# Pooled attention feeding two expert stages on one Trainium2 core: the order of the score chunks, the shape of the minimum over scores, and the visits of the product with v

## The chip, the cores and the metric

The kernel runs on one core of one Trainium2 chip. The metric is device time in microseconds (us). The core's engines work side by side and meet at semaphores: TensorE (PE in the profile, with its weight loads shown apart as PEld), VectorE (DVE), ScalarE (ACT), GpSimd (POOL) and SyncE (SP), which issues most of the transfers.

## The reference

Three parts follow each other. Only the first, attention, is touched by the change.

```python
q_pool = q.reshape(B, H, S // 2, 2, D).mean(axis=3)       # B, H, S, D = 4, 8, 1152, 64
scores = scale * np.matmul(q_pool, k.transpose(0, 1, 3, 2))
scores = scores - np.max(scores, axis=-1, keepdims=True)
attn = np.exp(scores)
attn = attn / (np.sum(attn, axis=-1, keepdims=True) + 1e-09)
attn_out = np.matmul(attn, v)                              # then to (B*S/2, H*D) = x
```

Then x goes through a soft mixture of 8 experts with 4 slots each (logits x @ phi, softmax over tokens and over slots, two products per expert with a relu between), and last through h = x @ w_in, (h - tanh(h)) @ w_out. All inputs and the output are float32.

## The kernel before

**Pairs, rounds and tiles.** The 32 heads are worked in 16 pairs (`over_pairs`; the first two and last two pairs are written out, the 12 between run in a hardware loop). A pair has 576 pooled query rows for each of its two heads. They make nine tiles of 128 rows in five rounds: rounds 0, 1, 3 and 4 work a tile of each head (double rounds), and round 2 (`MIX`) works one tile that holds the last 64 rows of both heads.

**A round.** `scores` makes the scores of a tile against 1152 keys in three chunks, of 512, 512 and 128 keys (chunks 0, 1, 2), in this order. Each chunk takes three products (high and low halves of split operands) for each head, and lies in PSUM bank 3 * head + chunk, so banks 0 to 5 hold a round's scores. Scores are made with a negative factor, so their minimum is the wanted maximum. On VectorE `maximum` takes it, head after head: a reduction over each 512-wide chunk, then one `tensor_scalar` with an accumulated minimum over the 128-wide chunk, which takes the two reduced values as scalars. ScalarE's `exponential` waits for that, and writes one probability row block of 1152 columns in one instruction. TensorE turns (transposes) it in nine 128-wide pieces (`turn_prob`), and ScalarE and VectorE copy the turned pieces to `probT` (`evac`). Head 0's turned chunks use banks 0, 1 and 2, head 1's use banks 6, 5 and 4. VectorE copies head 0's chunk 1 (`second_a`) and both heads' chunk 2 (`third_evac`); ScalarE copies both heads' chunk 0 (`first_evac`) and head 1's chunk 1 (`second_b`).

**The order on TensorE** in each round: the three chunks of scores, each behind the waits of `banks_free`; in round 2 also the turning of the next pair's k and q (`turn_k_and_q`); in rounds 1 and 3 the turning back of an output (`turn_out`); a visit of the product with v; the turning of head 0; perhaps a second visit; the turning of head 1. The product with v (`pv`) of a group of query tiles has 18 matmuls in the program, each of which shows as two in the profile. `PV_AT` gives each visit as (round, place): (group, pairs back, from, to). Group 0 has 320 columns and group 1 has 256.

**Round 2 to round 3.** Round 2 turns the next pair's k and q into banks 3 to 6. VectorE copies k out (`k_raw`, L432), ScalarE copies q out (`q_raw`, L500), and GpSimd makes the high and low parts. In the code before, ScalarE first copies chunk 0 of the mixed tile and then q. Round 3's first scores wait for chunk 0 of the mixed tile to be copied (`first_evac`) and for `k_copied`; its second chunk waits for `second_a` and `third_evac`; its third waits for `q_evac`.

**Downstream.** SyncE prefetches expert weights during the last pair; one of these transfers goes to memory that the attention's operands of the odd pairs use, so it waits for the last scores.

Of the kernel before, what the change touches and what calls it, by code (L numbers as in the profile page):

```python
# [10 lines left out]
P = 128  # L11
# [6 lines left out]
def attention(nc, dram, sizes, sb, x, ident, rep, rep_ready, rep_step, early, prefetch):  # L18
# [19 lines left out]
    def heads_of(r):  # L38
        return 1 if r == MIX else 2

    def tiles_of(p, r):

        return p * TILES + 2 * r - (1 if r > MIX else 0)
# [5 lines left out]
    def group_of(r):  # L49
# [3 lines left out]

    PV_AT = {(3, 0): (0, 0, 0, 8), (3, 1): (0, 0, 8, 10), (4, 0): (0, 0, 10, 18),
             (0, 0): (1, 1, 0, 10), (0, 1): (1, 1, 10, 12), (1, 0): (1, 1, 12, 18)}
    OUT_AT = {1: 0, 3: 1}
    PV_EVAC_AT = {0: 0, 2: 1}

    with ExitStack() as ctx:
# [19 lines left out]
        part_neg = sb("part_neg", [P, 2, 2])  # L79
        spare = sb("spare", [P, P])  # L80
        neg_max = sb("neg_max", [P, TILES])
# [55 lines left out]
        def _(sp):  # L137
# [33 lines left out]
            over_pairs(sp, body)  # L171
            sp.wait_ge(scores_full, PAIRS * ROUNDS * NCH)
            prefetch(sp, 2)
# [49 lines left out]
        def turned(h, c):  # L223

            n = (CHUNK[c][1] - CHUNK[c][0]) * P
            return ps[:, (c, (TBANK, 5, 4)[c])[h], 0:n]

        @block.tensor
        def _(pe):
# [27 lines left out]

            def banks_free(p, r, c, first, last):

                before = tiles_of(p, r)  # L260
                if c == 0:
                    wait(pe, first_evac, before - (0 if r == MIX + 1 else 1))
                    if r == MIX + 1 and not last:
                        pe.wait_ge(k_copied, p + 1)
                elif c == 1:
                    wait(pe, second_a, p * ROUNDS + r)
                    wait(pe, third_evac, before)
                elif r == MIX + 1 and not last:
                    pe.wait_ge(q_evac, p + 1)
                elif r != MIX:  # L270
                    wait(pe, second_b, doubles_of(p, r))

# [41 lines left out]
            def body(p, par, first, last):  # L314
                for r in range(ROUNDS):
                    for c in range(NCH):
                        banks_free(p, r, c, first, last)
                        if r == 0 and c == 0:
                            if first:
                                pe.wait_ge(first_kl, 1)  # L320
                                pe.wait_ge(first_ql, 1)
                            wait(pe, k_low, p)
                            wait(pe, q_low, p)
                        scores(p, par, r, c)

                    wait(pe, first_evac, tiles_of(p, r))
                    if r == MIX and not last:
                        wait(pe, second_b, doubles_of(p, r))
                        turn_q_rest(p + 1, ps[:, TBANK - 1, BANK - P:BANK])
                        turn_k_and_q(p + 1, q_row)  # L330
                    if r in OUT_AT and not first:
                        turn_out(p - 1, OUT_AT[r])
                    visit(p, par, r, 0, first)
                    turn_prob(p, r, 0)
                    visit(p, par, r, 1, first)
                    if r != MIX:
                        if r in OUT_AT and not first:
                            pe.wait_ge(out_evac, (p - 1) * 2 + OUT_AT[r] + 1)
                        turn_prob(p, r, 1)
# [6 lines left out]

            def visit(p, par, r, n, first):
                if (r, n) in PV_AT:
                    g, back, lo, hi = PV_AT[r, n]
                    if not (back and first):  # L350
                        pv(p - back, par ^ back, g, lo, hi)
# [21 lines left out]
        def _(dve):  # L373
# [7 lines left out]

            def maximum(p, r, h):

                tau = tiles_of(p, r) + h
                j = tiles_of(0, r) + h
                full = (p * ROUNDS + r) * NCH
                part = part_neg[:, h]
                wait(dve, neg_done, tau - 1)
                for c in range(2):
                    dve.wait_ge(scores_full, full + c + 1)  # L390
                    nc.vector.tensor_reduce(part[:, c:c + 1], ps[:, 3 * h + c, :], AX.X, ALU.min).then_inc(part_done, 1)  # L391
                dve.wait_ge(scores_full, full + NCH)
                dve.wait_ge(part_done, tau * 2 + 2)
                wait(dve, exp_done, tau - TILES + 1)
                nc.vector.tensor_scalar(spare[:], ps[:, 3 * h + 2, 0:P], part[:, 0:1], part[:, 1:2],  # L395
                                        ALU.min, ALU.min, accum_out=neg_max[:, j:j + 1]).then_inc(neg_done, 1)

            def invert(p, par):
# [21 lines left out]
            def body(p, par, first, last):  # L420
                for r in range(ROUNDS):
                    tau = tiles_of(p, r)
                    for h in range(heads_of(r)):
                        maximum(p, r, h)
                    if r == 0 and not first:
# [23 lines left out]
        def _(act):  # L449
# [35 lines left out]
            def body(p, par, first, last):  # L485
                for r in range(ROUNDS):
# [3 lines left out]
                    for h in range(heads_of(r)):  # L490
                        exponential(p, par, r, h)
                    group_free(act, p, r)
                    act.wait_ge(ptr_full, tau * NCH + 1)
                    evac(copy, r, 0, 0).then_inc(first_evac, 1)
                    if r == MIX:
                        if not last:
                            act.wait_ge(qtr_full, p + 2)
                            act.wait_ge(k_copied, p + 1)
                            wait(act, q_low, p)
                            nc.scalar.activation(q_raw[:], q_row, ACT.Copy, scale=EXP_SCALE).then_inc(q_evac, 1)  # L500
                    else:
                        act.wait_ge(ptr_full, tau * NCH + NCH + 1)
# [587 lines left out]
def program(nc, dram, out, sizes):  # L1090
# [9 lines left out]
    def rows(start, *items):  # L1100

        table = {}
        for name, size in items:
# [4 lines left out]
    KV, QT, QR = S // P, SQ // P, SQ % P  # L1108
    QC = 2 * QT * P + 3 * QR
    XW = B * H // 2 * (QT + 1) * P  # L1110
# [9 lines left out]
               ("q_both", 2 * QT * D), ("q_both_r", 2 * D), ("q_raw", SQ + QR)),  # L1120
        **rows(ODD, ("kT0", 2 * S), ("qT_hi0", QC), ("qT_lo0", QC)),
        **rows(EVEN, ("kT1", 2 * S), ("qT_hi1", QC), ("qT_lo1", QC)),
        **rows(TOP, ("v_nat0", 2 * KV * D), ("v_nat1", 2 * KV * D), ("prob0", S), ("prob1", S), ("probT0", G0W), ("probT1", G1W),
               ("outT0", 2 * P + QR), ("outT1", 2 * P), ("ones", 8), ("warm", 8), ("part_neg", 8), ("spare", P), ("neg_max", 16),
               ("row_sum0", 16), ("row_sum1", 16), ("mix_sum0", 8), ("mix_sum1", 8), ("row_den", 16), ("row_inv", 16)),
# [12 lines left out]
    TABLE = {**NEVER, **ATTENTION, **KEPT, **GATING, **EXPERTS}  # L1138
    assert KEPT["stand"] + 32 <= PT and GATING["xT1"] + KD * SQ * 4 <= PT and GATING["row"] + 16 * NT <= END + 2048
    assert max(GATING["dT"] + LW * 4, ATTENTION["row_inv"] + 64) <= nc.sbuf_usable_end - BASE  # L1140
# [90 lines left out]
```

## Time and profile before

| | |
|---|---|
| median of three runs | 919.76 us (919.64 to 921.55) |
| the profiled execution's own time | 917.36 us |
| its span in the profile | 915.6 us |
| attention | from the start to 584 us |
| weight transfers, gating and experts | 584 to about 680 us |
| last part (w_in, tanh, w_out) | about 680 us to the end |
| PE busy over the span | 817.7 us (89%) |
| DVE, ACT, POOL busy | 551.7 us, 487.3 us, 248.7 us |

The span is that of the recorded instructions; the rest of the own time, 1.8 us, lies around it. Matmuls are pipelined and the ends of their rows are modelled, so a busy PE isn't PE at its peak. What sets the pace of the attention is read from the order in time within one round.

### The profile page before, as it was taken

How to read it: one execution, taken by the hardware profiler on the slowest of the kernel's cores; microseconds unless marked ns; L12 is line 12 of the kernel's file. 1: busy time of each engine (PE TensorE's matmuls, PEld its weight loads, DVE VectorE, ACT ScalarE, POOL GpSimd, SP SyncE). 2: the span in 40 equal slices, each digit the busy share in tenths (PEclk: the TensorE clock that was granted, in tenths of full speed). 3: DMA queues.
4: the chain of work that ended last, by engine and by line, in shares of the span. 5: the costliest groups of instructions: out<-in, count | busy, mean ns of one | idle time of the engine just before them, and what ended most of it. 6: DMA issues, size and time to landing. Idle time of an engine off the chain costs nothing. (4 is left out here: it accounts for less than half of the span.)

```text
span 915.6 us, 16591 instructions
## 1 busy us (share of the span) xinstructions
PE 817.7 (89%) x5819; PEld 595.7 (65%) x5819; DVE 551.7 (60%) x1112; ACT 487.3 (53%) x729; POOL 248.7 (27%) x154
## 2 busy tenths in 40 slices
PE   4899899899899898898899898878578999999998
PEld 3666666666666666666666666544235888888886
DVE  3666666666766666667667666350007667766673
ACT  2555565555555555555655654321019666666662
POOL 2304304304214124124034030000008544443333
PEclk9999999999999999999999999989989999999999
DMA  5343203213113023023023061707990000000000
GB/s 129 140 126 78 61 20 78 48 30 77 30 48 77 15 63 77 1 76 77 0 77 78 1 236 67 276 2 291 395 401 15 24 24 23 23 23 23 23 22 24
DMA packets 82161, 75.50 MB, mean 82 GB/s; under 512 B 42448, under 2 KB 60880, under 8 KB 81616
## 3 DMA queue, kind: packets, MB, share of 16 engines
q1 hardware_dynamic: 79792, 74.47, 25.6%
q10 hardware_dynamic: 2336, 0.59, 0.3%
q8 instruction: 21, 0.34, 0.2%
q14 instruction: 12, 0.10, 0.0%
HBM read 70.32 MB, written 4.72 MB: 82 GB/s over the span
## 5 line engine op out<-in xcount | busy, mean ns | idle before, releaser
L478 ACT ACTIVATE prob<-ps,neg_max 128x1152 f32<-128x1152 f32 x144 | 175.8, 1221 | 213.4 <-DVE spare L395 213.4
L280 PE MATMUL ps<-ident,prob 128*128 128x128 f32 x1296 | 174.6, 281 | 51.4 <-ACT prob L478 49.9
L391 DVE TENSOR_REDUCE part_neg<-ps 128x1 f32<-128x512 f32 x288 | 191.8, 688 | 46.2 <-PE ps L254 37.3
L280 PEld LDWEIGHTS ps<-ident,prob 128*128 128x128 f32 x1296 | 140.8, 142 | 107.0 <-ACT prob L478 97.9
L296 PE MATMUL ps<-probT,v_nat 128*64 128x256 f32 (+1 forms) x1152 | 160.5, 414 | 0.0
L363 DVE COPY probT<-ps 128x128 f32<-128x128 f32 (+1 forms) x192 | 75.5, 421 | 101.9 <-PE ps L280 101.9
L451 ACT ACTIVATE probT<-ps 128x512 f32<-128x512 f32 x208 | 116.8, 593 | 33.8 <-PE ps L280 33.8
L208 POOL TENSOR_TENSOR kT<-k_raw,ones 128x1152 fp32r<-128x1152 f32 x15 | 31.6, 2107 | 342.4 <-DVE k_raw L432 342.4
L254 PE MATMUL ps<-kT,qT_hi 64*128 64x512 f32 (+1 forms) x768 | 111.7, 366 | 4.8 <-DVE qT_lo L380 2.6
L296 PEld LDWEIGHTS ps<-probT,v_nat 128*64 128x64 f32 x1152 | 74.5, 136 | 51.2 <-issue 10.9
L948 PE MATMUL ps<-w_hi,g_even 128*128 128x512 f32 x320 | 102.7, 392 | 2.2 <-POOL g_even L1032 2.0
L254 PEld LDWEIGHTS ps<-kT,qT_hi 64*128 64x128 f32 x768 | 68.8, 187 | 29.5 <-issue 7.8
L948 PE MATMUL ps<-w_hi,g_odd 128*128 128x512 f32 x256 | 81.7, 390 | 0.0
L1006 ACT ACTIVATE slot<-ps 128x1024 f32<-128x1024 f32 x36 | 37.0, 1028 | 64.7 <-PE ps L932 64.7
L948 PEld LDWEIGHTS ps<-w_hi,g_even 128*128 128x128 f32 x320 | 60.2, 188 | 15.7 <-POOL g_even L1032 2.9
L254 PE MATMUL ps<-kT,qT_lo 64*128 64x512 f32 (+1 forms) x384 | 69.6, 354 | 0.0
L395 DVE TENSOR_SCALAR_CACHE_REDUCE spare<-ps,part_neg 128x128 f32<-128x128 f32 x144 | 59.0, 409 | 17.1 <-DVE part_neg L391 0.6
L1071 DVE SCALAR_TENSOR_TENSOR slot<-slot,ps 128x1024 f32<-128x1024 f32 x36 | 44.0, 1222 | 38.7 <-ACT ps L1008 38.7
L1032 POOL TENSOR_TENSOR g_even<-slot,g_even 128x1024 fp32r<-128x1024 f32 x20 | 48.2, 2408 | 58.1 <-ACT g_even L993 58.1
L948 PE MATMUL ps<-w_lo,g_even 128*128 128x512 f32 x160 | 62.6, 391 | 0.0
L1078 DVE COPY_PREDICATED slot<-slot,ps 128x1024 f32<-128x1024 uint32 x36 | 49.3, 1368 | 21.9 <-DVE slot L1071 20.3
L948 PEld LDWEIGHTS ps<-w_hi,g_odd 128*128 128x128 f32 x256 | 48.2, 188 | 9.7
(142 smaller groups left out, 1002.9 us busy)
## 6 DMA issues: line engine op xcount, KB each, us to landing
slot<-in_moe_w SPq DMA_DIRECT2D x16, 2048.0 KB, 12.8
v_nat<-in_v SPq DMA_DIRECT2D x16, 576.0 KB, 4.8
k_nat<-in_k SPq DMA_DIRECT2D x30, 288.0 KB, 4.0
q_nat<-in_q SPq DMA_DIRECT2D x32, 256.0 KB, 4.2
out<-res SPq DMA_DIRECT2D x18, 256.0 KB, 2.0
slot<-in_moe_w_in SPq DMA_DIRECT2D x2, 2048.0 KB, 20.7
slot<-in_moe_w_out SPq DMA_DIRECT2D x8, 512.0 KB, 16.8
q_nat_r<-in_q SPq DMA_DIRECT2D x32, 32.0 KB, 3.6
```

The costliest lines, as they stand in the source:

```text
L254: last = nc.tensor.matmul(ps[:, 3 * h + c, 0:k1 - k0], q[par][HALF[h], at], kT[par][HALF[h], part, k0:k1], start=(n == 0), stop=(n == 2))
L280: last = nc.tensor.transpose(dst[:, n * P:(n + 1) * P], prob[h][:, kt * P:(kt + 1) * P], ident[:])
L296: last = nc.tensor.matmul(ps[64 * h:64 * h + D, VBANK, 0:n], v_nat[par][:, h, kt, :], probT[g][:, kt, h, :], start=(kt == 0), stop=(kt == ...
L363: return copy(probT[g][:, k0:k1, h, col:col + P], src.rearrange("p (c q) -> p c q", c=n))
L391: nc.vector.tensor_reduce(part[:, c:c + 1], ps[:, 3 * h + c, :], AX.X, ALU.min).then_inc(part_done, 1)
L395: nc.vector.tensor_scalar(spare[:], ps[:, 3 * h + 2, 0:P], part[:, 0:1], part[:, 1:2], ALU.min, ALU.min, accum_out=neg_max[:, j:j + 1]).th ...
L451: return nc.scalar.activation(dst, src, ACT.Copy)
L478: nc.scalar.activation(prob[h][:], row, ACT.Exp, bias=neg_max[:, j:j + 1], scale=-1.0, accum_out=sums).then_inc(exp_done, 1)
L948: last = nc.tensor.matmul(ps[:, 2 * HB + i, :], a[par][:, ft * CW + i * P:ft * CW + (i + 1) * P], w(ft), start=(ft == 0 and k == 0), stop= ...
L1032: nc.gpsimd.tensor_tensor(g_block(g_lo, par, b), g[b % 2], g_block(g_hi, par, b).bitcast(F32), ALU.subtract).then_inc(gl_done, 1)
L1071: nc.vector.scalar_tensor_tensor(tv[b % 2], sq[b % 2], 1.0, h_of(b), ALU.subtract, ALU.mult).then_inc(series_done, 1)
L1078: nc.vector.copy_predicated(tv[b % 2], big[b % 2].bitcast(mybir.dt.uint32), th).then_inc(tanh_done, 1)
```

## The change

The short chunk of the scores is made first, before the two wide ones (`SCORE_ORDER`). On VectorE the minimum of a double round becomes: one short reduction for each head over its 128-wide chunk, one reduction over head 0's chunk 0, one `tensor_scalar` with accumulated minimum over head 0's chunk 1, and one over head 1's chunks 0 and 1 together, 1024 columns. The mixed tile has the same without the second head. Head 1's turned chunks 1 and 2 move from banks 5 and 4 to banks 4 and 3, and the waits of `banks_free` follow the new order and banks. In round 2 ScalarE copies q out before chunk 0 of the mixed tile. The product with v has four visits instead of six: what was between the two turnings goes ahead of the first. One prefetch waits for the last minimum instead of the last scores. The scratch output `spare` becomes two tensors, of 512 and 1024 columns, and the memory map is changed for it.

```diff
-    PV_AT = {(3, 0): (0, 0, 0, 8), (3, 1): (0, 0, 8, 10), (4, 0): (0, 0, 10, 18),
-             (0, 0): (1, 1, 0, 10), (0, 1): (1, 1, 10, 12), (1, 0): (1, 1, 12, 18)}
+    PV_AT = {3: (0, 0, 0, 10), 4: (0, 0, 10, 18), 0: (1, 1, 0, 10), 1: (1, 1, 10, 18)}
+    SCORE_ORDER = (2, 0, 1)
...
-            sp.wait_ge(scores_full, PAIRS * ROUNDS * NCH)
+            sp.wait_ge(neg_done, PAIRS * TILES)
             prefetch(sp, 2)
...
-            return ps[:, (c, (TBANK, 5, 4)[c])[h], 0:n]
+            return ps[:, (c, (TBANK, 4, 3)[c])[h], 0:n]
...
-            def banks_free(p, r, c, first, last):
-
-                before = tiles_of(p, r)
-                if c == 0:
-                    wait(pe, first_evac, before - (0 if r == MIX + 1 else 1))
+            def banks_free(p, r, c, last):
+
+                done = tiles_of(p, r)
+                firsts = done - (0 if r == MIX + 1 else 1)
+                if c == 2:
+                    wait(pe, third_evac, firsts)
+                    if r == MIX + 1 and not last:
+                        pe.wait_ge(q_evac, p + 1)
+                elif c == 0:
+                    wait(pe, first_evac, firsts)
                     if r == MIX + 1 and not last:
                         pe.wait_ge(k_copied, p + 1)
-                elif c == 1:
+                    elif r != MIX:
+                        wait(pe, third_evac, done)
+                else:
                     wait(pe, second_a, p * ROUNDS + r)
-                    wait(pe, third_evac, before)
-                elif r == MIX + 1 and not last:
-                    pe.wait_ge(q_evac, p + 1)
-                elif r != MIX:
-                    wait(pe, second_b, doubles_of(p, r))
+                    if r != MIX:
+                        wait(pe, second_b, doubles_of(p, r))
...
-                    for c in range(NCH):
-                        banks_free(p, r, c, first, last)
+                    for c in SCORE_ORDER:
+                        banks_free(p, r, c, last)
...
                         wait(pe, second_b, doubles_of(p, r))
+                        wait(pe, third_evac, tiles_of(p, r))
                         turn_q_rest(p + 1, ps[:, TBANK - 1, BANK - P:BANK])
...
-                    visit(p, par, r, 0, first)
+                    visit(p, par, r, first)
                     turn_prob(p, r, 0)
-                    visit(p, par, r, 1, first)
...
-            def maximum(p, r, h):
+            def small(p, r, h, c, slot):
+
+                dve.wait_ge(scores_full, (p * ROUNDS + r) * NCH + SCORE_ORDER.index(c) + 1)
+                nc.vector.tensor_reduce(part_neg[:, h, slot:slot + 1], ps[:, 3 * h + c, 0:(CHUNK[c][1] - CHUNK[c][0]) * P],
+                                        AX.X, ALU.min).then_inc(part_done, 1)
+
+            def smallest(p, r, h, c0, c1, parts, slot):
 
                 tau = tiles_of(p, r) + h
                 j = tiles_of(0, r) + h
-                full = (p * ROUNDS + r) * NCH
-                part = part_neg[:, h]
-                wait(dve, neg_done, tau - 1)
-                for c in range(2):
-                    dve.wait_ge(scores_full, full + c + 1)
-                    nc.vector.tensor_reduce(part[:, c:c + 1], ps[:, 3 * h + c, :], AX.X, ALU.min).then_inc(part_done, 1)
-                dve.wait_ge(scores_full, full + NCH)
-                dve.wait_ge(part_done, tau * 2 + 2)
+                dve.wait_ge(scores_full, (p * ROUNDS + r) * NCH + NCH)
+                dve.wait_ge(part_done, parts)
                 wait(dve, exp_done, tau - TILES + 1)
-                nc.vector.tensor_scalar(spare[:], ps[:, 3 * h + 2, 0:P], part[:, 0:1], part[:, 1:2],
+                row = flat[:, (3 * h + c0) * BANK:(3 * h + c1) * BANK]
+                nc.vector.tensor_scalar(spare[h][:], row, part_neg[:, h, 0:1], part_neg[:, h, slot:slot + 1],
                                         ALU.min, ALU.min, accum_out=neg_max[:, j:j + 1]).then_inc(neg_done, 1)
+
+            def minima(p, r):
+
+                wait(dve, neg_done, tiles_of(p, r))
+                parts = p * (3 * ROUNDS - 1) + 3 * r - (1 if r > MIX else 0)
+                for h in range(heads_of(r)):
+                    small(p, r, h, 2, 0)
+                small(p, r, 0, 0, 1)
+                smallest(p, r, 0, 1, 2, parts + heads_of(r) + 1, 1)
+                if r != MIX:
+                    smallest(p, r, 1, 0, 2, parts + heads_of(r) + 1, 0)
...
                         exponential(p, par, r, h)
+                    if r == MIX and not last:
+                        act.wait_ge(qtr_full, p + 2)
+                        act.wait_ge(k_copied, p + 1)
+                        wait(act, q_low, p)
+                        nc.scalar.activation(q_raw[:], q_row, ACT.Copy, scale=EXP_SCALE).then_inc(q_evac, 1)
                     group_free(act, p, r)
                     act.wait_ge(ptr_full, tau * NCH + 1)
                     evac(copy, r, 0, 0).then_inc(first_evac, 1)
-                    if r == MIX:
-                        if not last:
-                            act.wait_ge(qtr_full, p + 2)
-                            act.wait_ge(k_copied, p + 1)
-                            wait(act, q_low, p)
-                            nc.scalar.activation(q_raw[:], q_row, ACT.Copy, scale=EXP_SCALE).then_inc(q_evac, 1)
-                    else:
+                    if r != MIX:
```

## Rows read from the trace of the kernel before

**Rows 1.** The page: granted clock in 40 slices, and transfers (KB each, us to landing)

```profile
PEclk9999999999999999999999999989989999999999
...
slot<-in_moe_w SPq DMA_DIRECT2D x16, 2048.0 KB, 12.8
```

**Rows 2.** Timeline: first weight load of each round of a pair (start us, us)

```profile
297.07 0.30 PEld L254 LDWEIGHTS ps<-kT,qT_hi 64*128 64x128 f32 x4 [0.17 <-issue]
...
304.39 0.30 PEld L254 LDWEIGHTS ps<-kT,qT_hi 64*128 64x128 f32 x4 [0.17 <-issue]
...
311.52 0.30 PEld L251 LDWEIGHTS ps<-kT,qT_hi 128*128 128x128 f32 x2
...
317.39 0.30 PEld L254 LDWEIGHTS ps<-kT,qT_hi 64*128 64x128 f32 x4 [0.38 <-ACT probT L451]
...
325.01 0.30 PEld L254 LDWEIGHTS ps<-kT,qT_hi 64*128 64x128 f32 x4 [0.17 <-issue]
...
332.13 0.30 PEld L254 LDWEIGHTS ps<-kT,qT_hi 64*128 64x128 f32 x4 [0.17 <-issue]
```

**Rows 3.** Timeline of round 4, from its second weight loads to the next round

```profile
326.03 1.38 DVE L391 TENSOR_REDUCE part_neg<-ps 128x1 f32<-128x512 f32 x2 [0.61 <-PE ps L254]
...
326.28 0.42 PEld L254 LDWEIGHTS ps<-kT,qT_hi 64*128 64x128 f32 x4
...
326.88 1.81 PEld L296 LDWEIGHTS ps<-probT,v_nat 128*64 128x64 f32 x16
...
327.44 0.41 DVE L395 TENSOR_SCALAR_CACHE_REDUCE spare<-ps,part_neg 128x128 f32<-128x128 f32 x1
...
327.78 1.28 DVE L391 TENSOR_REDUCE part_neg<-ps 128x1 f32<-128x512 f32 x2
327.98 1.22 ACT L478 ACTIVATE prob<-ps,neg_max 128x1152 f32<-128x1152 f32 x1 [2.31 <-DVE spare L395]
...
329.10 0.41 DVE L395 TENSOR_SCALAR_CACHE_REDUCE spare<-ps,part_neg 128x128 f32<-128x128 f32 x1
329.34 0.97 PEld L280 LDWEIGHTS ps<-ident,prob 128*128 128x128 f32 x9 [0.64 <-ACT prob L478]
...
329.63 1.22 ACT L478 ACTIVATE prob<-ps,neg_max 128x1152 f32<-128x1152 f32 x1 [0.34 <-DVE spare L395]
...
331.00 0.96 PEld L280 LDWEIGHTS ps<-ident,prob 128*128 128x128 f32 x9 [0.69 <-ACT prob L478]
...
332.24 0.29 DVE L363 COPY probT<-ps 128x128 f32<-128x128 f32 x1 [0.88 <-PE ps L280]
```

**Rows 4.** Timeline of round 1, the two ends of its minima

```profile
306.93 0.41 DVE L395 TENSOR_SCALAR_CACHE_REDUCE spare<-ps,part_neg 128x128 f32<-128x128 f32 x1
...
309.22 1.22 ACT L478 ACTIVATE prob<-ps,neg_max 128x1152 f32<-128x1152 f32 x1 [0.45 <-DVE spare L395]
```

**Rows 5.** Timeline of rounds 2 and 3

```profile
314.07 0.41 DVE L395 TENSOR_SCALAR_CACHE_REDUCE spare<-ps,part_neg 128x128 f32<-128x128 f32 x1
...
317.18 0.89 DVE L361 COPY probT<-ps 128x512 f32<-128x512 f32 x2 [1.18 <-PE ps L280]
...
318.18 0.33 PEld L254 LDWEIGHTS ps<-kT,qT_hi 64*128 64x128 f32 x4 [0.26 <-DVE probT L361]
...
319.75 1.81 PEld L296 LDWEIGHTS ps<-probT,v_nat 128*64 128x64 f32 x16 [0.17 <-issue]
...
322.06 0.96 PEld L280 LDWEIGHTS ps<-ident,prob 128*128 128x128 f32 x9 [0.49 <-ACT prob L478]
...
323.88 0.97 PEld L280 LDWEIGHTS ps<-ident,prob 128*128 128x128 f32 x9 [0.49 <-ACT prob L478]
```

**Rows 6.** VectorE's groups with shapes kept apart, 20 to 600 us (busy us, mean ns)

```profile
L395 DVE TENSOR_SCALAR_CACHE_REDUCE spare<-ps,part_neg 128x128 f32<-128x128 f32 x143 | 58.6, 409 | 17.0 <-DVE part_neg L391 0.6
...
L363 DVE COPY probT<-ps 128x128 f32<-128x128 f32 x128 | 36.6, 286 | 60.8 <-PE ps L280 60.8
L432 DVE COPY k_raw<-ps 128x1152 f32<-128x1152 f32 x15 | 20.4, 1358 | 2.3 <-PE ps L234 1.1
```

More of the change, by code:

```diff
@@ L79, in attention @@
         part_neg = sb("part_neg", [P, 2, 2])
-        spare = sb("spare", [P, P])
+        spare = [sb(f"spare{h}", [P, (h + 1) * BANK]) for h in range(2)]
         neg_max = sb("neg_max", [P, TILES])
@@ L315, in body @@
                 for r in range(ROUNDS):
-                    for c in range(NCH):
-                        banks_free(p, r, c, first, last)
-                        if r == 0 and c == 0:
+                    for c in SCORE_ORDER:
+                        banks_free(p, r, c, last)
+                        if r == 0 and c == SCORE_ORDER[0]:
                             if first:
@@ L345, in body, with visit @@
                     turn_out(p, 1)
-            def visit(p, par, r, n, first):
-                if (r, n) in PV_AT:
-                    g, back, lo, hi = PV_AT[r, n]
+            def visit(p, par, r, first):
+                if r in PV_AT:
+                    g, back, lo, hi = PV_AT[r]
                     if not (back and first):
@@ L422, in body @@
                     tau = tiles_of(p, r)
-                    for h in range(heads_of(r)):
-                        maximum(p, r, h)
+                    minima(p, r)
                     if r == 0 and not first:
@@ L1108, in program @@
     KV, QT, QR = S // P, SQ // P, SQ % P
-    QC = 2 * QT * P + 3 * QR
+    QC, BOTH_Q = 2 * QT * P + 3 * QR, (QT + 1) * P
     XW = B * H // 2 * (QT + 1) * P
@@ L1120, in program @@
                ("q_both", 2 * QT * D), ("q_both_r", 2 * D), ("q_raw", SQ + QR)),
-        **rows(ODD, ("kT0", 2 * S), ("qT_hi0", QC), ("qT_lo0", QC)),
-        **rows(EVEN, ("kT1", 2 * S), ("qT_hi1", QC), ("qT_lo1", QC)),
+        **rows(ODD, ("kT0", 2 * S), ("qT_hi0", BOTH_Q), ("qT_lo0", BOTH_Q)),
+        **rows(EVEN, ("kT1", 2 * S), ("qT_hi1", BOTH_Q), ("qT_lo1", BOTH_Q), ("spare1", 2 * BANK)),
         **rows(TOP, ("v_nat0", 2 * KV * D), ("v_nat1", 2 * KV * D), ("prob0", S), ("prob1", S), ("probT0", G0W), ("probT1", G1W),
-               ("outT0", 2 * P + QR), ("outT1", 2 * P), ("ones", 8), ("warm", 8), ("part_neg", 8), ("spare", P), ("neg_max", 16),
+               ("outT0", 2 * P + QR), ("outT1", 2 * P), ("ones", 8), ("warm", 8), ("part_neg", 8), ("spare0", BANK), ("neg_max", 16),
                ("row_sum0", 16), ("row_sum1", 16), ("mix_sum0", 8), ("mix_sum1", 8), ("row_den", 16), ("row_inv", 16)),
@@ L1138, in program @@
     TABLE = {**NEVER, **ATTENTION, **KEPT, **GATING, **EXPERTS}
-    assert KEPT["stand"] + 32 <= PT and GATING["xT1"] + KD * SQ * 4 <= PT and GATING["row"] + 16 * NT <= END + 2048
+    assert ATTENTION["spare1"] + 2 * BANK * 4 <= TOP and KEPT["stand"] + 32 <= PT and GATING["xT1"] + KD * SQ * 4 <= PT and GATING["row"] + 16 * NT <= END + 2048
     assert max(GATING["dT"] + LW * 4, ATTENTION["row_inv"] + 64) <= nc.sbuf_usable_end - BASE
```

## The prediction

> **What bounds the kernel now.** I read the page first: TensorE is at its full granted clock through the attention (a slice at 0.9 or more is all that the digits show there) [rows 1], so no stretch of it is explained by the clock. Shares of busy time don't say what a round waits for: TensorE is busy for 89% and yet stands before every turning. So I took the timeline of one pair from the hardware loop. The first weight loads of its rounds stand at 297.07, 304.39, 311.52, 317.39, 325.01 and 332.13 [rows 2]: rounds 0 to 4 take 7.32, 7.13, 5.87, 7.62 and 7.12, a pair 35.06 us. Sixteen such pairs make 561 of the 584 us of the attention. All that comes later hangs on its end, so what a pair wins or loses counts sixteen times.
>
> Then round 4, step by step from its start at 325.01 [rows 2, 3]: VectorE gets the first chunk at 1.02; two reductions; head 0's minimum starts at 2.43; two more reductions; head 1's minimum starts at 4.09; its exponential at 4.62; its turning at 5.99; the next round at 7.12. Each step starts when the one before ends, and head 0's exponential and turning (2.97, 4.33) lie beside. So a double round is bound by scores, six VectorE instructions, one exponential and one turning. The product with v fills TensorE's waiting. Rounds 0 and 1 are the same with some 0.1 us more ahead of each minimum (round 1: minimum at 306.93, which is 2.54 after its start; head 1's exponential at 4.83) [rows 2, 4].
>
> Round 3 differs. After 16 passes of the product with v (319.75 to 322.06, 0.144 each) the turning of head 0 starts at once, and after four more passes that of head 1, at 323.88 [rows 5]; both exponentials are done by then. TensorE itself bounds that round, and its length is what TensorE has to do from the moment its banks are free.
>
> **Part 1, the order of scores.** The short chunk of a double round takes six matmuls. Its weight loads start at 326.28, those of the next work at 326.88 [rows 3]: 0.60, of which up to a quarter is waiting for a matmul of the wide chunk before. Four loads at a round's start are busy for 0.30 together [rows 2] though the four of the last chunk take 0.42, so the heads' loads overlap. I put three steps of load, about 0.11 each, at 0.32, with 0.60 as the upper bound and as the lower 0.2, the time of two of the three steps. But chunk 0 now has another limit. Its bank 3 holds head 1's turned short piece. VectorE starts that copy 0.11 after the round's start and takes 0.29 [rows 3], so it ends at 0.40, and TensorE picks up 0.07 to 0.11 later: in round 3 the copies that start at 317.18 and take 0.89 end at 318.07, and the waiting load starts at 318.18 [rows 5]. Chunk 0 starts at 0.47, whatever the short chunk costs below that. The two short reductions fall in the gap before it. Chunk 0 reaches VectorE at 0.47 + 1.02 = 1.49, chunk 1 one pitch of 0.69 later, at 2.18.
>
> **Part 2, the minimum.** No row shows an accumulated minimum over more than 128 columns: that one takes 0.409 [rows 6]. Copies from PSUM give the cost of a column: (1.358 - 0.286) / 1024 = 1.047 ns [rows 6], over a bank's border too, and the reduction over 512 (0.69) has a like cost. So I take 0.409 + 0.40 = 0.81 for 512 columns and 0.409 + 0.94 = 1.35 for 1024. Bounds for the latter: no less than 0.94, its columns alone; no more than 2.29, if the accumulating form needs two steps for each column. I take the value by the single step, since the 128-wide form is only 0.12 above a 128-wide copy, which is below one further step of 128 columns.
>
> Round 4 then: reduction over head 0's chunk 0 from 1.49 to 2.18; minimum at 2.21; head 0's exponential as long behind it as now (0.54) plus 0.40: 3.15. Head 1's minimum follows head 0's by today's pitch 0.34 + 0.40, at 2.95. Its exponential comes 0.53 + 0.94 behind: 4.42. ScalarE is free (3.15 + 1.22 = 4.37). Turning 1.37 on at 5.79, next round 1.13 on: 6.92. Gain **0.20** against 7.12. TensorE's other work fits: scores and 16 passes end at 0.15 + 1.87 + 2.3 = 4.32, head 0's turning can start at 3.15 + 1.36 = 4.51.
>
> Rounds 0 and 1 have 0.1 more ahead of head 0's minimum (2.31) and no such pause ahead of head 1's, whose waits are worked through while head 0's instruction runs. Head 1's exponential then is due at 2.31 + 0.74 + 1.47 = 4.52, against 4.83 now: gains of **0.31** and, as in round 1 ScalarE is free only at 4.56, **0.27**. Three double rounds: 0.78 a pair.
>
> **Part 3, rounds 2 and 3.** In the mixed round chunk 0 comes 0.32 later and one reduction of 0.69 is gone, so the minimum starts at about 2.15 instead of 2.55 (314.07) [rows 2, 5]; it is 0.40 longer; the exponential starts as now. The k copy behind it waits for TensorE anyway. ScalarE's copy of q now lies ahead of that of chunk 0, in the time in which it waits for the turning; both end as now.
>
> Round 3's first work, the short chunk, needs bank 2, which holds the mixed tile's last turned piece. That copy ends at 318.07 and the load follows at 318.18, where the wide chunk 0 now starts at 317.39 [rows 2, 5]. TensorE has nothing else there: the next instructions in its queue are these. Before, 1.57 us lay between 318.18 and the product with v, for two chunks and the turned output. Now a third chunk of 0.69 goes in: 320.44. Then 20 passes instead of 16: 2.88, head 0's turning at 323.32. Before, 1.82 lay between the turnings, with four passes (0.58) and a switch of operand shape back and forth (the issue gap of 0.17); without them 1.05: 324.37. Next round at 325.50 or, with the switch not saved twice, 325.4 to 325.7. Loss **0.43** against 325.01, within 0.35 to 0.65. The exponentials don't bind: by the sum above head 1's would let its turning start at 323.9.
>
> **Part 4, the visits.** In rounds 0, 1 and 4 the passes moved ahead of head 0's turning lie in time in which TensorE waits: in round 1, 16 passes of at most 0.13 end at 2.5 + 2.1 = 4.6, head 0's turning is due at 4.7. Price without that cover: up to 0.1. **The prefetch** (2048 KB, 12.8 us to landing [rows 1]) is issued some 3 us later, from the last scores to the last minimum of the last pair; behind it two more. The expert that uses them starts after the whole gating stage: nothing. Memory layout and written-out pairs: nothing of their own.
>
> **Sum.** -0.78 + 0.43 = -0.35 a pair, times 16 = -5.6 us. From the profiled execution's own 917.4 that is 911.8; the median of the runs lies 2.4 above, so against it I say **914.2**.
>
> Two rules of the Trainium skill bear on it. "VectorE: DVE Perf Modes", the section on the TRN2 errata, gives a PSUM-source instruction 120 cycles plus one for each column: an estimate of 1.19 us for 1024 columns and 0.26 for 128. The trace has 0.409 for the latter [rows 6], so the fixed part here is larger, and I keep the row's; by the page each double round would gain up to 0.3 more. "TensorE: Matmul & The Clock Gate", section "Back-to-back issue gap", speaks against the change: short matmuls don't go at the rate of their columns, 128-wide ones take about 81 ns each with their loads, where 512-wide take 131. By it six short ones cost 0.49 where nothing longer covers them. In double rounds the wait to 0.47 hides that; rounds 2 and 3 would lose some 0.2 more, and the sum would be about -2.6 us.
>
> **Rivals.**
> - *The minima gain nothing that the new wait doesn't eat.* Place: chunk 0 of each double round, behind the copy of head 1's short piece. It is the last VectorE copy of the old round, so it is now in the chain. If chunk 0 starts at 0.59 instead of 0.47 (0.60 is the upper bound of the short chunk) the doubles gain 0.42 and round 3 takes it back: 919.8 on the median's scale. For it: the hand-over at 318.18 took 0.11 [rows 5], and 0.60 for the short chunk isn't excluded. Against: TensorE's wait for this copy is a single one.
> - *Slower: wide accumulated minima cost more than their columns.* Place: both L395 successors. With an excess e on 1024 columns and e/2 on 512, head 1's exponential is late by 1.5 e. It eats the 0.35 of a pair at e = 0.08, and from e = 0.10 the kernel is slower by over 0.2%. At e = 0.3 a pair loses 1.0, 935; at two steps a column (e = 0.94) it loses over 4, past 980. For it: no row has the form at that width. Against: the 128-wide form's small excess over a copy.
> - *Slower by the hand-over alone*: the same wait as in the first rival, at a higher price. From chunk 0 at 0.63 on the kernel is slower by over 0.2%. At 0.70, that is 0.3 from the end of the copy to the first wide load, three double rounds lose 0.69 of their 0.78, round 3 takes its 0.43: +0.34 a pair, 919.8 + 5.4 = 925. Against: no hand-over in the rows is above 0.11.
>
> **How the numbers follow.** Forecast 0.58. No change 0.19. The slow minimum 0.12, the slow hand-over 0.11. A difference of 0.2% (1.8 us) is about what a measurement of this kernel can tell from none. Faster 0.58, same 0.19, slower 0.23. The range reaches from 909 (the doubles gain 0.1 more each) to 923, which takes in no change and most of the slow hand-over, and leaves out the slow minimum.
>
> **What would show it.** In double rounds the first wide reduction at 1.5 after the start, head 1's exponential at 4.4 to 4.6, rounds of 6.9 to 7.0. One accumulated minimum of 1.35 and one of 0.81. In round 3 a start that waits for VectorE's L361 successor, 0.8 later than now, and a length of about 7.3. The forecast is wrong if the 1024-wide instruction is over 1.45, or if chunk 0 starts later than 0.6, or if rounds 2 and 3 together grow by more than 0.8.

## The result and the profile after

The changed kernel takes 933.7 us against 919.7 (medians of four runs each): ratio 1.0159, 95% interval 1.0131 to 1.0187. It is slower by 14 to 15 us, where 914.2 had been forecast. Its profiled execution took 933.6 us, with a span of 931.8.

The page first: TensorE's clock, in tenths of full speed.

```profile
PEclk9999999999999999999999998888979999999999
```

The slices of the attention up to 559 us still show a 9, which is 0.90 or more: a page of 40 slices can hide a short stretch at the lower clock. But the mean granted clock has gone from 0.988 to 0.967. The next four slices read 8, where [rows 1] have a 9 in three of the four; the first of them, 559 to 582 us, still lies in the attention.

The timeline of one pair from the hardware loop: the first weight load of each round (start, us), the turning of the mixed tile with the copy behind it, and the loads of the wide chunk in round 3:

```profile
301.03 0.30 PEld L254 LDWEIGHTS ps<-kT,qT_hi 64*128 64x128 f32 x4 [0.17 <-issue]
...
308.17 0.30 PEld L254 LDWEIGHTS ps<-kT,qT_hi 64*128 64x128 f32 x4 [0.17 <-issue]
...
315.12 0.30 PEld L251 LDWEIGHTS ps<-kT,qT_hi 128*128 128x128 f32 x2
...
319.72 1.20 PE L284 MATMUL ps<-ident,prob 128*128 128x128 f32 x9 [1.08 <-ACT prob L493]
...
320.85 0.89 DVE L365 COPY probT<-ps 128x512 f32<-128x512 f32 x2 [1.25 <-PE ps L284]
321.79 0.30 PEld L254 LDWEIGHTS ps<-kT,qT_hi 64*128 64x128 f32 x4 [1.11 <-DVE probT L365]
321.79 0.44 PE L254 MATMUL ps<-kT,qT_hi 64*128 64x128 f32 x4 [0.87 <-DVE probT L365]
...
322.12 0.30 PEld L254 LDWEIGHTS ps<-kT,qT_hi 64*128 64x128 f32 x4
...
329.02 0.30 PEld L254 LDWEIGHTS ps<-kT,qT_hi 64*128 64x128 f32 x4 [0.17 <-DVE probT L367]
...
336.15 0.30 PEld L254 LDWEIGHTS ps<-kT,qT_hi 64*128 64x128 f32 x4 [0.17 <-issue]
```

Rounds 0 to 4 take 7.14, 6.95, 6.67, 7.23 and 7.13, a pair 35.12 us. In [rows 2] it was 7.32, 7.13, 5.87, 7.62 and 7.12, 35.06 together. So this pair has gained 0.18, 0.18 and nothing in its double rounds 0, 1 and 4 and lost 0.41 in rounds 2 and 3, and hardly differs. Sixteen such pairs would be 1 us slower.

TensorE stands idle twice around the turning of the mixed tile: 1.08 us ahead of it and 0.87 behind it. In the same pair of the kernel before the first wait is there, and the scores of round 3 begin 0.14 us after the turning's end (317.39):

```profile
316.05 1.20 PE L280 MATMUL ps<-ident,prob 128*128 128x128 f32 x9 [1.01 <-ACT prob L478]
```

Not all pairs are like that. In the same profile, two pairs on, round 3 starts at 392.07 and the next at 400.85: 8.78 instead of 7.23. The two cases side by side (stretch, us; busy time of each engine; then granted clock, DMA share, GB/s):

```profile
core 0: us, PE busy (x) PEld busy (x) DVE busy (x) ACT busy (x) POOL busy (x), PEclk, DMA share, GB/s
...
320.80:321.80 1.00, 0.13 (x4) 0.01 (x2) 0.89 (x2) 0.21 (x1) 1.00 (x1) 1.00 0.08 1
321.80:329.00 7.20, 7.20 (x58) 4.87 (x58) 4.49 (x10) 3.53 (x6) 5.74 (x5) 1.00 0.86 227
...
391.10:392.10 1.00, 0.13 (x3) 0.03 (x2) 0.89 (x2) 0.18 (x1) 1.00 (x1) 1.00 0.08 1
392.10:395.50 3.40, 3.40 (x19) 2.38 (x20) 1.18 (x3) 0.00 (x0) 3.32 (x3) 0.53 0.79 175
```

Both come behind the same wait. In the second the granted clock falls from 2.4 to 1.2 GHz right behind it, and the scores of round 3, which TensorE itself bounds, take 3.32 us instead of 1.91. Such rounds 3, of 8.4 to 8.8 us, stand in six of the first fifteen pairs of this profile, and there is one more stretch at 1.2 GHz, longer, in the last pair. The kernel before has none in the attention. Seven times 1.55 us is 10.9 us. The stage behind the attention is hit too: its first 19.6 us, at 1.00 in the kernel before, are at

```profile
595.40:615.00 19.60, 19.26 (x156) 13.92 (x156) 6.11 (x11) 4.62 (x8) 1.81 (x1) 0.74 0.43 164
```

and from the end of the attention to the last part some 5 us are lost. With the 1 us from above this makes, within 1 us, the 16.2 between the two profiled spans (931.8 and 915.6; the profiled execution of the kernel before was one of its faster ones, so the medians are 2 us closer).

Last the steps of round 4, as in [rows 3], and the new minimum's two forms (busy us, mean ns):

```profile
329.54 0.33 PEld L254 LDWEIGHTS ps<-kT,qT_hi 64*128 64x128 f32 x4
...
330.57 0.69 DVE L389 TENSOR_REDUCE part_neg<-ps 128x1 f32<-128x512 f32 x1 [0.46 <-PE ps L254]
...
331.45 0.81 DVE L400 TENSOR_SCALAR_CACHE_REDUCE spare<-ps,part_neg 128x512 f32<-128x512 f32 x1 [0.19 <-DVE part_neg L389]
...
332.19 1.34 DVE L400 TENSOR_SCALAR_CACHE_REDUCE spare<-ps,part_neg 128x1024 f32<-128x1024 f32 x1
...
333.65 1.22 ACT L493 ACTIVATE prob<-ps,neg_max 128x1152 f32<-128x1152 f32 x1
...
335.01 0.96 PEld L284 LDWEIGHTS ps<-ident,prob 128*128 128x128 f32 x9 [0.30 <-ACT prob L493]
```

```profile
L400 DVE TENSOR_SCALAR_CACHE_REDUCE spare<-ps,part_neg 128x1024 f32<-128x1024 f32 x64 | 85.9, 1342 | 0.0
...
L400 DVE TENSOR_SCALAR_CACHE_REDUCE spare<-ps,part_neg 128x512 f32<-128x512 f32 x79 | 64.0, 810 | 17.6 <-DVE part_neg L389 10.9 <-PE ps L254 4.9
```

From the start at 329.02: wide chunk's loads at 0.52, reduction at 1.55, head 0's minimum at 2.43, head 1's at 3.17, its exponential at 4.63, its turning at 5.99. The last is the number of the kernel before.

The pairs that are written out, outside the hardware loop, look better: in pair 1 (counted from 0) only 0.11 lie between the reduction and the minimum, where the loop has 0.19, and in pairs 1 and 14 the rounds 0, 1 and 4 are 0.19 to 0.25 shorter than in the kernel before. So part of that pause goes with the loop.

### The profile page after: what moved, and what is told of

It is laid out like the page before. It is cut to its first block and busy times, and to the rows that moved or that the text cites. A ratio compares the mean times of both kernels' runs of the same rounds, so it can differ in the third digit from the quotient of the medians.

```text
span 931.8 us, 16526 instructions
## 1 busy us (share of the span) xinstructions
PE 840.6 (90%) x5819; PEld 609.3 (65%) x5819; DVE 542.4 (58%) x1048; ACT 485.7 (52%) x729; POOL 248.9 (27%) x154
## 5 line engine op out<-in xcount | busy, mean ns | idle before, releaser
L284 PE MATMUL ps<-ident,prob 128*128 128x128 f32 x1296 | 171.2, 280 | 34.3 <-ACT prob L493 32.2
L400 DVE TENSOR_SCALAR_CACHE_REDUCE spare<-ps,part_neg 128x1024 f32<-128x1024 f32 (+1 forms) x144 | 145.9, 1046 | 18.2 <-DVE part_neg L389 10.9
L300 PE MATMUL ps<-probT,v_nat 128*64 128x256 f32 (+1 forms) x1152 | 154.3, 413 | 0.0
L254 PE MATMUL ps<-kT,qT_hi 64*128 64x512 f32 (+1 forms) x768 | 123.5, 397 | 16.4 <-DVE probT L365 13.8
L389 DVE TENSOR_REDUCE part_neg<-ps 128x1 f32<-128x128 f32 (+1 forms) x224 | 91.3, 431 | 60.7 <-PE ps L254 53.5
L300 PEld LDWEIGHTS ps<-probT,v_nat 128*64 128x64 f32 x1152 | 77.5, 137 | 62.7 <-issue 18.4
L254 PEld LDWEIGHTS ps<-kT,qT_hi 64*128 64x128 f32 x768 | 71.8, 199 | 37.3 <-DVE probT L365 17.8
L254 PE MATMUL ps<-kT,qT_lo 64*128 64x512 f32 (+1 forms) x384 | 75.9, 375 | 0.0
```

What stands on the lines that cost most here:

```text
L254: last = nc.tensor.matmul(ps[:, 3 * h + c, 0:k1 - k0], q[par][HALF[h], at], kT[par][HALF[h], part, k0:k1], start=(n == 0), stop=(n == 2))
L284: last = nc.tensor.transpose(dst[:, n * P:(n + 1) * P], prob[h][:, kt * P:(kt + 1) * P], ident[:])
L300: last = nc.tensor.matmul(ps[64 * h:64 * h + D, VBANK, 0:n], v_nat[par][:, h, kt, :], probT[g][:, kt, h, :], start=(kt == 0), stop=(kt == ...
L389: nc.vector.tensor_reduce(part_neg[:, h, slot:slot + 1], ps[:, 3 * h + c, 0:(CHUNK[c][1] - CHUNK[c][0]) * P], AX.X, ALU.min).then_inc(part ...
L400: nc.vector.tensor_scalar(spare[h][:], row, part_neg[:, h, 0:1], part_neg[:, h, slot:slot + 1], ALU.min, ALU.min, accum_out=neg_max[:, j:j ...
```

## The experiments

**The filler.** The first theory to test was the clock: is it the cause or a bystander?

```diff
+            def filler(n):
+                for _ in range(n):
+                    nc.tensor.transpose(ps[:, VBANK, 0:P], ident[:], ident[:])
...
                     visit(p, par, r, first)
+                    if r == MIX and not last:
+                        wait(pe, pv_evac, p * 2)
+                        filler(8)
                     turn_prob(p, r, 0)
+                    if r == MIX and not last:
+                        filler(6)
```

> The changed kernel with turnings of the identity matrix, whose result nobody reads, put into TensorE's two waits of the mixed round: 8 ahead of the mixed tile's turning and 6 behind it (they go to bank 7, which is free there). My theory (the clock): what makes the change slower are stretches at 1.2 GHz that begin after the long waits around the mixed tile's turning, seven of them in the attention and a longer one after it. Then filled waits leave no stretch at the lower clock in rounds 3 of the first 15 pairs, rounds of 7.2 us there, and a time of 919 to 924 us, 10 to 15 below the changed kernel. Rival (the waits themselves): the added wait of round 3 costs its own length and the clock is a bystander. Then the time stays at 932 to 935, or rises by what the filler overlaps.

Measured: 921.6 us (ten runs, 917.9 to 930.1), ratio 1.0025 (1.0001 to 1.0049). TensorE does more, and the kernel is 12 us faster than the changed one. In the profiled execution (930.1, the longest of the ten) all rounds 3 of the first fifteen pairs take 6.9 to 7.3 us; its stretches at the lower clock lie in rounds 0 and 1 of the first pair, in the last pair, which has no filler, and behind it. Behind the attention alone it loses 8 us against the kernel before. So the loss there doesn't need the stretches in rounds 3, and what brings it stays open. Then each of the two waits alone:

> The changed kernel with the filler only in the wait ahead of the mixed tile's turning (1.08 us in the changed kernel's profile). If the lower clock needs both waits, no stretch at 1.2 GHz in rounds 3 of the loop and 919 to 925 us. If the wait behind the turning, which the change adds, is enough by itself: stretches as in the changed kernel and 931 to 935 us.

> The changed kernel with the filler only in the wait behind the mixed tile's turning, the one that the change adds (0.87 us). The wait ahead of the turning is in the kernel before too (1.01 us), which shows no stretch at 1.2 GHz in the attention. So none here, and 919 to 925 us, of which the length of the added wait remains.

Measured: 920.0 us with the first wait filled (eight runs, 918.9 to 929.3; ratio 1.0037, 1.0002 to 1.0071) and 919.5 with the second (915.9 to 921.8; ratio 1.0002, 0.9982 to 1.0022). Either is enough for rounds 3: none of 8.8 us in the first fifteen pairs of either profile (6.9 to 7.3). But three of the eight runs with the first wait filled took 927.7 to 929.3 us, at a mean granted clock of 0.967 to 0.972; they have no timeline, so where they lost the time isn't known. With the second filled all eight are at 0.976 or more. The timeline with the second filled:

```profile
316.32 0.97 PEld L289 LDWEIGHTS ps<-ident,prob 128*128 128x128 f32 x9 [1.31 <-ACT prob L503]
...
317.36 0.82 PE L280 MATMUL ps<-ident 128*128 128x128 f32 x6
...
318.40 0.30 PEld L254 LDWEIGHTS ps<-kT,qT_hi 64*128 64x128 f32 x4 [0.46 <-DVE probT L375]
```

The wait still has its length; only TensorE isn't idle in it. What is left of the change, without the clock, is no difference.

**The wait alone.** The other way round: the kernel before, with the wait that the change brings.

```diff
                     if r == MIX + 1 and not last:
                         pe.wait_ge(k_copied, p + 1)
+                    if r == MIX + 1:
+                        wait(pe, third_evac, before)
```

> The kernel before with one wait more: round 3's first chunk also waits for the copy of the mixed tile's last turned piece, as the change makes it wait. The clock theory: round 3 starts 0.7 to 0.8 later in each pair (11 to 13 us in all, little of it won back), and stretches at 1.2 GHz turn up in some rounds 3 at about 1.5 us each: 935 to 945 us. Rival (the wait costs only its length): 930 to 932 and a granted clock as before.

Measured: 936.4 us (936.1 to 937.9), ratio 1.0183 (1.0159 to 1.0207). One wait in the old kernel makes it slower than the whole change did. Its round 2 takes 6.66 instead of 5.87, and three rounds 3, in pairs 1 to 3, take 9.06 instead of 7.53. One of them, over its first 3.2 us:

```profile
74.00:77.20 3.20, 3.20 (x20) 2.57 (x16) 1.38 (x2) 0.00 (x0) 3.20 (x2) 0.55 0.93 213
```

So the wait costs nearly its length in every pair (0.79 in round 2, of which round 3 gives 0.10 back: 11 us in sixteen) and now and then a stretch at 1.2 GHz: three times 1.53, and a longer one in the last pair. In this kernel the first is most of it. The other twelve pairs have the same two waits (1.01 and 0.96 in a pair of the loop) and keep the clock. So the two waits don't bring the lower clock each time, and what picks the pairs stays open.

**Round 3 in the old order.** The changed kernel with the wait taken away, by making round 3's wide chunks first.

```diff
+    def order_of(r):
+        return (0, 1, 2) if r == MIX + 1 else SCORE_ORDER
...
-                    for c in SCORE_ORDER:
+                    for c in order_of(r):
...
+                if r == MIX + 1:
+                    small(p, r, 0, 0, 1)
                 for h in range(heads_of(r)):
                     small(p, r, h, 2, 0)
-                small(p, r, 0, 0, 1)
+                if r != MIX + 1:
+                    small(p, r, 0, 0, 1)
```

> The changed kernel, but round 3 makes its chunks in the old order (0, 1, 2), with VectorE's minima in the order that suits it; everything else as changed. The clock theory: round 3 starts as early as in the kernel before, no stretch at 1.2 GHz in the attention, and rounds 0 and 1 keep their gain of 0.18 each: 0.35 to 0.5 a pair under the kernel before, 912 to 916 us. Rival (the new order as such is bad, in the double rounds too): 920 or more.

Measured: 907.2 us (six runs), ratio 0.9875 (0.9842 to 0.9908): 12 to 13 us faster than the kernel before and 26 faster than the changed one, more than was expected.

```profile
305.47 0.30 PEld L254 LDWEIGHTS ps<-kT,qT_hi 128*128 128x128 f32 x2
...
310.07 1.20 PE L287 MATMUL ps<-ident,prob 128*128 128x128 f32 x9 [1.08 <-ACT prob L499]
...
311.42 0.30 PEld L257 LDWEIGHTS ps<-kT,qT_hi 64*128 64x128 f32 x4 [0.38 <-ACT probT L472]
...
318.66 0.30 PEld L257 LDWEIGHTS ps<-kT,qT_hi 64*128 64x128 f32 x4 [0.17 <-DVE probT L370]
```

Round 2 takes 5.95 here, and round 3 7.24, with 7.23 to 7.27 in all of the first fifteen pairs. The wait of 1.08 ahead of the turning is as in the changed kernel, but no second one follows, and the clock stays in them. The last pair has a stretch at 1.2 GHz here too (549.5 to 552.9, granted clock 0.50), as it has with the visits alone (556.4 to 559.8), where neither order nor minimum is changed: the second wait isn't what brings that one. The sum against the changed kernel: 0.73 less in sixteen pairs is 11.7 us, six stretches fewer are 9.3, the shorter one in the last pair is 1.4, and the stage behind loses nearly 5 less. That is 1 us more than the 26 between the spans; the written-out pairs differ by less than 0.73.

**The other parts apart.** First the visits.

```diff
-    PV_AT = {(3, 0): (0, 0, 0, 8), (3, 1): (0, 0, 8, 10), (4, 0): (0, 0, 10, 18),
-             (0, 0): (1, 1, 0, 10), (0, 1): (1, 1, 10, 12), (1, 0): (1, 1, 12, 18)}
+    PV_AT = {(3, 0): (0, 0, 0, 10), (4, 0): (0, 0, 10, 18),
+             (0, 0): (1, 1, 0, 10), (1, 0): (1, 1, 10, 18)}
```

> The kernel before with the four visits of the product with v and nothing else changed. If the visits are free in rounds 0, 1 and 4 and save round 3 a switch of operand shape, 916 to 919.5 us, rounds 3 of about 7.45 instead of 7.63. If the idle time that they open between the turnings brings the lower clock: some stretches at 1.2 GHz and 922 or more.

Measured: 915.5 us, ratio 0.9951 (0.9933 to 0.9969).

```profile
315.24 0.30 PEld L254 LDWEIGHTS ps<-kT,qT_hi 64*128 64x128 f32 x4 [0.38 <-ACT probT L451]
...
317.60 2.35 PEld L296 LDWEIGHTS ps<-probT,v_nat 128*64 128x64 f32 x20 [0.17 <-issue]
...
320.45 1.99 PEld L280 LDWEIGHTS ps<-ident,prob 128*128 128x128 f32 x18 [0.49 <-issue]
...
322.60 0.30 PEld L254 LDWEIGHTS ps<-kT,qT_hi 64*128 64x128 f32 x4 [0.17 <-issue]
```

Both turnings of round 3 now run as one row of 18, and the round takes 7.36 instead of 7.62. The other rounds of the loop are unchanged to 0.01. Sixteen times 0.26 is 4.2 us, of the 4.5 between the medians.

Then order and minimum, each with the visits but without the other.

```diff
-                    minima(p, r)
+                    for h in range(heads_of(r)):
+                        maximum(p, r, h)
```

> The kernel of e1_round3_old_order with the minimum of the kernel before (two wide reductions and a short accumulated minimum for each head), so the new order of scores in rounds 0, 1, 2 and 4 without its minimum. My theory: in the double rounds the new order makes the first wide chunk some 0.5 us later (it waits for the copy of head 1's short piece and comes behind the short chunk), and only the new minimum, which finds the short chunks done, takes that back. Then rounds 0, 1 and 4 take 0.3 to 0.5 us more than in the kernel before: 935 to 942 us. Rival (the order is worth something by itself): under 915.5, the time with the four visits alone.

Measured: 945.7 us, ratio 1.0289 (1.0268 to 1.0310), above what was expected. Rounds 0, 1 and 4 take 7.86, 7.66 and 7.65: 0.53 more than before in each. The row that shows why, in a round that starts at 317.25:

```profile
317.77 0.33 PEld L257 LDWEIGHTS ps<-kT,qT_hi 64*128 64x128 f32 x4
...
318.80 1.38 DVE L398 TENSOR_REDUCE part_neg<-ps 128x1 f32<-128x512 f32 x2 [1.15 <-PE ps L257]
```

The first wide chunk is ready at 1.55 instead of 1.02, and all behind it is as late.

> The kernel before with the four visits and the new minimum, but the old order of scores in all rounds (VectorE reduces head 0's first chunk, then the two short ones). My theory: the short chunks are there only at 2.0 us after the round's start, the two short reductions lie on the path in place of one wide one, and head 1's exponential comes at about 4.9 us: rounds 0 and 1 as before, round 4 slower by 0.2 to 0.3: 918 to 923 us. Rival (the merged minimum is what gains, the order doesn't matter): 907 to 910.

This is the kernel before with the visits of the diff above, the later prefetch and the new `minima`, whose short reductions come after head 0's wide one. Measured: 922.8 us, ratio 1.0039 (1.0026 to 1.0052). Rounds 0 and 1 as before, round 4 0.19 slower, round 2 0.28 slower:

```profile
328.76 0.69 DVE L385 TENSOR_REDUCE part_neg<-ps 128x1 f32<-128x512 f32 x1 [0.60 <-PE ps L254]
...
329.73 0.49 DVE L385 TENSOR_REDUCE part_neg<-ps 128x1 f32<-128x128 f32 x2 [0.28 <-PE ps L254]
```

VectorE waits 0.28 for the short chunks and then works 0.49 on the path. Beside the visits alone (915.5), the order costs 30 us, the minimum 7, and both together, with round 3 in the old order, gain 8: each of them pays only with the other.

**The pause ahead of the minimum.** Three waits stand ahead of it; the last to be fulfilled was put last. Built on the kernel of round 3 in the old order.

```diff
+                wait(dve, exp_done, tau - TILES + 1)
                 dve.wait_ge(scores_full, (p * ROUNDS + r) * NCH + NCH)
                 dve.wait_ge(part_done, parts)
-                wait(dve, exp_done, tau - TILES + 1)
```

> The kernel of e1_round3_old_order with the three waits ahead of each accumulated minimum in another order: the one on the exponential of nine tiles ago, long fulfilled, first, then the scores, and the one on VectorE's own reductions last. In the changed kernel 0.19 us lie between the end of the wide reduction and head 0's minimum, where my prediction had 0.03. Theory (the pause is the working through of waits that come behind the scores' one): it falls to 0.05 to 0.1, rounds 0, 1 and 4 get shorter by about 0.1 each, 4 to 7 us off: 900 to 903. Rival (the pause is the hand-over of the reduction's own signal): no change, 906 to 908.

Measured: 905.2 us (six runs: four of 903.3 to 906.1, two of 914.9), ratio 0.9884 (0.9841 to 0.9928). In the profile (903.3) the rounds 0, 1 and 4 of the loop take 7.06, 6.86 and 7.05, 0.08 less than without it:

```profile
324.56 0.69 DVE L392 TENSOR_REDUCE part_neg<-ps 128x1 f32<-128x512 f32 x1 [0.48 <-PE ps L257]
...
325.37 0.81 DVE L403 TENSOR_SCALAR_CACHE_REDUCE spare<-ps,part_neg 128x512 f32<-128x512 f32 x1
```

From the reduction's end at 325.25 to the minimum 0.12 are left of 0.19. The profile confirms part of the theory, and the gain is in the loop alone: a pair there is 0.38 shorter, the written-out pairs 1 and 14 are 0.17 longer. The median lies above the 900 to 903 that were expected; in the whole kernel, with intervals that overlap, it can't be told from 907.2.

**The changed kernel again.**

> The changed kernel again, unaltered, on the chip of this set: 932 to 936 us and, in its profile, rounds 3 of two kinds, 7.2 and 8.8 us. Were the low-clock stretches a matter of chance, they would fall in other rounds or be another number.

Measured: 933.4 us (930.7 to 934.0), ratio 1.0145 (1.0122 to 1.0167). The profile has six rounds 3 of 8.8 us in the first fifteen pairs, as many as the first profile, and one more stretch in the last pair, as before. The pairs hit are 1, 3, 8, 10, 12 and 14, where they were 0, 3, 5, 10, 12 and 14: four are the same, and from pair 10 on it is every second one in both. That isn't even chance; what it follows stays open.

## Why the prediction was wrong

**The step that failed is the first sentence of the reading**: "so no stretch of it is explained by the clock". It was true of the kernel before, and I took it for a property of the stage. That put the clock's cost at nothing without a reason. The sum had no term for the clock, no rival had one, and so the range ended at 923. The change put a second idle wait of TensorE, 0.87, 1.2 us behind one of 1.08. The kernel before has the first (1.01) and not the second, and keeps its clock; the second with the first filled keeps it in rounds 3 too; both together lose it in six of the first fifteen pairs of the changed kernel, and in three of them in the kernel before with the wait added. Filling either takes 14 us off, filling both 12. That the two waits together bring the lower clock of rounds 3 is shown by these pairs of kernels; for the stretch in the last pair and for the stage behind it isn't. None of the signs of being wrong that I had named was met: the 1024-wide instruction took 1.342, chunk 0 started at 0.52, rounds 2 and 3 grew by 0.41. All were about lengths at the full clock. The Trainium skill, "TensorE: Matmul & The Clock Gate", in "HAM oscillation", describes a kernel in which each wait of some 3 to 5 us for a transfer, between bursts of matmuls, brings the clock down. The trace agrees that waits do it, but here two much shorter ones, 1.08 and 0.87 us with 1.2 us of work between them, were enough in some pairs.

**Rounds 2 and 3**: the mechanism and the size were right. Predicted +0.43 (the steps that I wrote down end at 325.50 and make 0.49), measured +0.41 in the pairs with the full clock: round 3's start waits for the copy of the mixed tile's last piece (320.85 + 0.89 = 321.74, load at 321.79). The short chunk costs 0.33 there (321.79 to 322.12; I had 0.32). The 0.49 that I worked out from the Trainium skill, "TensorE: Matmul & The Clock Gate", section "Back-to-back issue gap", isn't borne out.

**The double rounds**: right in mechanism, too large in size. Predicted gains 0.31, 0.27 and 0.20, measured 0.18, 0.18 and 0. Two terms. The wide chunk's loads start at 0.52 instead of 0.47, and it reaches VectorE at 1.55 instead of 1.49. And between reduction and minimum I had 0.03 in round 4 from [rows 3], where the new code has 0.19, in rounds 0 and 1 0.20 instead of 0.10 to 0.14. Together they put head 0's minimum at 2.43, just where it was before, and head 1's exponential 0.21 later than forecast. Of the pause the turned waits took back 0.07, and in written-out pair 1 of the changed kernel it is 0.08 shorter than in the loop; what the rest is stays open.

**The price of wide minima** was right: 0.810 and 1.342 against 0.81 and 1.35. The rival of a slow minimum falls. The estimate of 1.19 for 1024 columns, worked out from the section on the TRN2 errata of "VectorE: DVE Perf Modes" in the Trainium skill, is too low here, as it was for 128. **The rivals of the hand-over** fall too: it took 0.05 more than the forecast, not the 0.16 that was needed for a slower kernel. **The visits** gained their switch of operand shape in round 3, which my sum held, and cost nothing elsewhere. **The later prefetch** wasn't tried by itself.

With the clock left out my sum would have been 0.06 instead of -0.35 a pair. So of the 19.5 us between forecast and result some 6.6 are the 0.41 a pair, nearly all of it the double rounds, and the other 13 the clock, which fits the 12 to 14 that the fillers take off.

## What to carry to other kernels

Where a chain bound by hand-overs leaves TensorE idle, look at how the idle pieces lie to each other before moving a wait: a new one close behind another can cost more by the clock than by its length, and only a narrow window behind the waits shows where, not the row of digits on the page. A few matmuls whose result nobody reads, in one of the waits, are a cheap test, and so is the wait alone in the old kernel. When a reordering is right in most rounds, look for the one round whose first resource comes free last, and leave it its own order: here that is the difference between 1.6% slower and 1.2% faster.

## What the runs showed of the hardware

Two idle waits of 1.08 and 0.87 us on either side of 1.2 us of turnings were followed in six of the first fifteen pairs by a stretch at 1.2 GHz that made round 3 about 1.55 us longer, though the engine was busy from the second wait on. Waits of about the same length in the other kernel (1.01 and 0.96) were followed by one in three of fifteen. With turnings that nobody reads in one of the waits (eight in 1.04 us or six in 0.82) no round 3 of the first fifteen pairs was hit. The pairs hit differ between two profiles of one kernel; their number is six in both, with one more stretch in the last pair, and the eight times of the changed kernel, 930.7 to 935.5 us, differ by 0.5% at most.
